# Attention, gated FFN and top-1 experts on one core: softmax steps reordered, PV in two runs, first FFN blocks between attention's last steps

## What is computed

```python
# attention: 4 batches x 8 heads, 576 tokens, head size 64, fp32
scores = 0.125 * q @ k.T                  # masked block-causally, blocks of 64 tokens
attn   = exp(scores - max) ; attn /= attn.sum(-1) + 1e-9
x = (attn @ v), heads side by side        # 2304 x 512
# gated FFN, 512 -> 1536 -> 512
y = (sigmoid(x @ w_gate) * (x @ w_val)) @ w_out
# top-1 of 8 experts, 512 -> 1024 -> 512
out[t] = gate[t] * relu(y[t] @ w1[e]) @ w2[e],  e = argmax(y[t] @ wr)
```

## Time and profile before

| | |
|---|---|
| median of 3 runs | 988.29 us (987.73 to 992.08) |
| profiled execution | 989.87 us, its span 988.2 us |
| busy | PE 914.9 us (93%), DVE 338.4 (34%), ACT 298.7 (30%), POOL 253.3 (26%) |
| attention stage | 5.3 us to 213.0 us; a pair takes about 12.6 us |
| mean granted TensorE clock | 0.973 of full speed |
| DMA sizes, median us from issue to landing | w1raw 768 KB, 5.5; kt and qt 288 KB each, 3.5 and 4.0; rwide 144 KB in two issues, 2.9; xo store 288 KB, 3.1; rinv store 4.5 KB, 2.7; xraw 768 KB, 4.6 |

### The profile page before, as it was taken

One profiled execution on the slowest core, in us unless ns is written; L12 is line 12 of the kernel. 1 busy time (PEld: TensorE's weight loads), 2 busy tenths in 40 slices (PEclk: granted clock), 3 DMA queues, 4 the chain that ended last, 5 costly groups with the idle time before them and its releaser, 6 DMA issues.

```text
span 988.2 us, 15746 instructions
## 1 busy us (share of the span) xinstructions
PE 914.9 (93%) x5370; PEld 758.9 (77%) x5371; DVE 338.4 (34%) x635; ACT 298.7 (30%) x654; POOL 253.3 (26%) x249
## 2 busy tenths in 40 slices
PE   6888888889999999999999999999379998999995
PEld 3444444469999999999999999998268887888884
DVE  5666666652210200210110120112663444235421
ACT  4555454433222212112112112112253354134310
POOL 4033333312211111111111111111444344225421
PEclk9999999999999999999999999999599999999998
DMA  4444444333110100000010000000373556116310
GB/s 131 152 153 153 136 135 147 124 122 107 43 43 33 33 1 32 6 27 32 1 32 32 1 1 11 23 2 32 138 260 132 190 181 226 42 43 220 114 42 29
DMA packets 45536, 83.08 MB, mean 84 GB/s; under 512 B 6831, under 2 KB 19119, under 8 KB 45488
## 3 DMA queue, kind: packets, MB, share of 16 engines
q1 hardware_dynamic: 39728, 67.21, 20.9%
q0 software_dynamic: 3360, 10.49, 3.1%
q10 hardware_dynamic: 2400, 4.72, 1.3%
HBM read 68.17 MB, written 14.75 MB: 84 GB/s over the span
## 4 chain that ended last, share of the span: by engine, by line
PE 85%; DVE 4%; issue 3%; POOL 2%; DMA 2%; ACT 2%; ACTq 0%; DVEq 0%; SPq 0%; POOLq 0%
PE bank L1163 22%; PE bank L1165 22%; PE bank L1164 22%; PE bank L1130 6%; PE bank L1103 5%; PE bank L1091 4%; DVE nmax L842 2%; PE bank L1300 2%; DMA stage<-in_we 2%; PE bank L1222 1%; POOL ew1l L368 1%; ACT prob L672 1%; PE bank L1213 1%; PE bank L1274 1%; DVE xo L821 1%
## 5 line engine op out<-in xcount | busy, mean ns | idle before, releaser
L1163 PE MATMUL bank<-xh,w1h 128*128 128x384 f32 x576 | 196.0, 340 | 0.0
L1165 PE MATMUL bank<-xh,w1l 128*128 128x384 f32 x576 | 193.2, 335 | 0.0
L1164 PE MATMUL bank<-xl,w1h 128*128 128x384 f32 x576 | 193.1, 335 | 0.0
L573 POOL TENSOR_TENSOR hl<-hraw,hh 128x384 fp32r<-128x384 f32 x72 | 77.2, 1072 | 399.1 <-ACT hh L701 399.1
L890 DVE TENSOR_TENSOR hraw<-sig,bank 128x384 f32<-128x384 f32 x72 | 39.9, 555 | 340.8 <-ACT sig L730 340.7
L730 ACT ACTIVATE sig<-bank 128x384 f32<-128x384 f32 x72 | 35.4, 492 | 259.5 <-PE bank L1165 259.5
L1163 PEld LDWEIGHTS bank<-xh,w1h 128*128 128x128 f32 x576 | 108.3, 188 | 1.8
L1164 PEld LDWEIGHTS bank<-xl,w1h 128*128 128x128 f32 x576 | 108.3, 188 | 1.7
L672 ACT ACTIVATE prob<-bank,nmax 128x576 f32<-128x576 f32 (+2 forms) x144 | 76.3, 531 | 105.5 <-DVE nmax L842 88.3
L1165 PEld LDWEIGHTS bank<-xh,w1l 128*128 128x128 f32 x576 | 108.1, 188 | 0.0
L1091 PE MATMUL bank<-kt,qt 64*64 64x64 f32 (+7 forms) x640 | 71.5, 441 | 16.6 <-ACT prob L672 11.3
(11 more groups left out here) (147 smaller groups left out, 1299.6 us busy)
## 6 DMA issues: line engine op xcount, KB each, us to landing
stage<-in_we SPq DMA_DIRECT2D x56, 512.0 KB
w1raw<-in_w SPq DMA_DIRECT2D x8, 768.0 KB, 5.5
kt<-in_kT SPq DMA_DIRECT2D x16, 288.0 KB, 3.5
qt<-in_qT SPq DMA_DIRECT2D x16, 288.0 KB, 4.0
rwide<-rinv_scratch SPq DMA_DIRECT2D x32, 144.0 KB, 2.9
xt_scratch<-xo SPq DMA_DIRECT2D x16, 288.0 KB, 3.1
xraw<-xt_scratch SPq DMA_DIRECT2D x6, 768.0 KB, 4.6
y_scratch<-yrow ACTq DMA_DIRECT2D x6, 768.0 KB, 3.6
```

The costliest lines, as they stand in the source:

```text
L573: pool.tensor_tensor(hl[:, f % 2, :], hraw[:, f % 2, :], hh[:, f % 2, :].bitcast(F32), ALU.subtract).then_inc(h_low, 1)
L1163: pe.matmul(out_, wh, ah, start=first, stop=False, skip_group_check=True)
L1164: pe.matmul(out_, wh, al, start=False, stop=False, skip_group_check=True)
L1165: return pe.matmul(out_, wl, ah, start=False, stop=last, skip_group_check=True)
```

## The change

1. **DVE's order in a pair.** Copies stand in a table (`OUT_V`). The maximum of step 0 comes ahead of the copy of the last pair's u6; the copy of u8 stays behind maximum 1; `recips` is one step earlier (step 1); `o_out` moves from step 1, where it did pair g-2, to step 8, where it does pair g-1.
2. **ACT's order** (`OUT_A`). The copy of the last pair's u9 comes ahead of exponential 2 and no longer behind it.
3. **PE.** PV's parts at steps 6 and 8 become one run at step 6.
4. **SP.** `o_store(g-2)` moves behind the v loads (ahead of `w1raw`); the first `xraw` load moves ahead of the last batch's pairs; the wait for the last `xo` store ahead of the `w_out` loads is gone.
5. **POOL** splits the first x in the last batch (`x_split`); ACT and DVE no longer do.
6. **Handover.** PE does `turn` of u6 and u7, then `up(0,0,0)`, then u8, u9, PV, and `up(0,0,1)`. The last `o_out` comes behind the first `hraw`. The last batch is written out behind the loop on all engines.

```diff
-        LAG, PE_LAG = 3, 4
+        PE_LAG = 4
+        OUT_V = {0: (1, 5), 1: (1, 7), 3: (0, 0), 4: (0, 1), 5: (0, 2), 6: (0, 3)}
+        OUT_A = {0: (1, 6), 2: (1, 8), 3: (0, 0), 7: (0, 4)}
-        PV_STEP = {4: [0], 6: [1, 2], 8: [3, 4]}
-        RSUM_STEP, O_STEP = 2, 1
+        PV_STEP = {4: [0], 6: [1, 2, 3, 4]}
+        RSUM_STEP, O_STEP = 1, 8
...
@@ SP, pair @@
                 if not early:
-                    if p == 3:
-                        o_store(b, 0)
-                    elif not isinstance(b, int):
-                        o_store(b - 1, p + 1)
                     rinv_store(g - 2, p % 2)
                     rwide_load(g - 2, p % 2)
                     sp.wait_ge(pv_done, g - 1)
...
+                if p >= 2:
+                    o_store(b, p - 2)
+                elif not (isinstance(b, int) and b == 0):
+                    o_store(b - 1, p + 2)
...
             xload(0, PPB)
-            o_store(BATCH - 1, PPB - 3)
+            for p in range(PPB):
+                pair(BATCH - 1, p)
...
-            o_store(BATCH - 1, PPB - 1)
             sp.wait_ge(pv_done, NPAIR)
-            sp.wait_ge(w1_low, 2 * C)
-            for i in range(2):
-                sp.wait_ge(xo_stored[i], 16 * NPAIR // 2)
+            sp.wait_ge(scores_done, NB * NPAIR)
             for k in range(FC):
+                if k == 2:
+                    o_store(BATCH - 1, PPB - 1)
...
@@ ACT, pair @@
+                    if i == 2 and not start:
+                        after_unit(g - 1, p - 1, OUT_A[i][1])
                     act.wait_ge(nmax_done, n + 1)
...
-                    if i >= LAG:
-                        after_unit(g, p, i - LAG)
-                    elif not start:
-                        after_unit(g - 1, p - 1, i + NB - LAG)
+                    if i != 2 and i in OUT_A and not (start and OUT_A[i][0]):
+                        back, j = OUT_A[i]
+                        after_unit(g - back, p - back, j)
...
@@ DVE, pair @@
+                    if i in OUT_V and not (start and OUT_V[i][0]):
+                        back, j = OUT_V[i]
+                        after_unit(g - back, p - back, j)
                     if i == RSUM_STEP and not start:
                         recips(g - 1, (p - 1) % 2)
...
-                    if i == O_STEP and not (isinstance(b, int) and g < 2):
-                        o_out(g - 2, p % 2)
+                    if i == O_STEP and not start:
+                        o_out(g - 1, (p - 1) % 2)
...
@@ PE, end of attention @@
+            turn(NPAIR - 1, PPB - 1, NB - 4)
+            turn(NPAIR - 1, PPB - 1, NB - 3)
+            pe.wait_ge(exp_done, NB * NPAIR - 2)
+            up(0, 0, 0)
+            turn(NPAIR - 1, PPB - 1, NB - 2)
+            turn(NPAIR - 1, PPB - 1, NB - 1)
+            pv(NPAIR - 1, PPB - 1, list(range(KT_N)))
+            pe.wait_ge(exp_done, NB * NPAIR)
+            up(0, 0, 1)
             group(0, 0)
```

More of the change, by code:

```diff
@@ L124, in bass_attention_ffn_moe @@
         wol = sb(s2, "wol", [P, FC, D], F32R)
+        woraw = sb(s2, "woraw", [P, 2, D])
         xh.append(sb(s2, "xh1", [P, C, GT], F32R))
         xl.append(sb(s2, "xl1", [P, C, GT], F32R))
-        woraw = sb(s2, "woraw", [P, 2, D])
         yrow = sb(s2, "yrow", [P, GM, D])
@@ L452, in _ @@
             sp.dma_start(wr_sb[:], wr.rearrange("(c p) e -> p c e", p=P)).then_inc(wr_loaded, 16)
-            with sp.Fori(1, BATCH) as b:
+            with sp.Fori(1, BATCH - 1) as b:
                 for p in range(PPB):
@@ L547, in w1_split, with x_split @@
                                    ALU.subtract).then_inc(w1_low, 1)
+            def x_split():
+                pool.wait_ge(x_loaded, 16)
+                pool.tensor_copy(xh[0][:].rearrange("p c n -> p (c n)"), xraw[:].rearrange("p c n -> p (c n)")
+                                 ).then_inc(x_high, 1)
+                pool.wait_ge(x_high, 1)
+                pool.tensor_tensor(xl[0][:].rearrange("p c n -> p (c n)"), xraw[:].rearrange("p c n -> p (c n)"),
+                                   xh[0][:].rearrange("p c n -> p (c n)").bitcast(F32), ALU.subtract
+                                   ).then_inc(x_low, 1)
             def pair(b, p):
@@ L557, in pair @@
                     w1_split(2 * b)
-                elif p == 0 and not isinstance(b, int):
+                elif p == 0 and not (isinstance(b, int) and b == 0):
                     w1_split(2 * b - 1)
+                elif p == 1 and isinstance(b, int) and b == BATCH - 1:
+                    x_split()
             for p in range(PPB):
                 pair(0, p)
-            with pool.Fori(1, BATCH) as b:
+            with pool.Fori(1, BATCH - 1) as b:
                 for p in range(PPB):
                     pair(b, p)
+            for p in range(PPB):
+                pair(BATCH - 1, p)
             w1_split(2 * C - 1)
@@ L674, in pair @@
                                    ).then_inc(exp_done, 1)
-                    if i >= LAG:
-                        after_unit(g, p, i - LAG)
-                    elif not start:
-                        after_unit(g - 1, p - 1, i + NB - LAG)
+                    if i != 2 and i in OUT_A and not (start and OUT_A[i][0]):
+                        back, j = OUT_A[i]
+                        after_unit(g - back, p - back, j)
             for p in range(PPB):
                 pair(0, p)
-            with act.Fori(1, BATCH) as b:
+            with act.Fori(1, BATCH - 1) as b:
                 for p in range(PPB):
                     pair(b, p)
+            for p in range(PPB):
+                pair(BATCH - 1, p)
             def xhigh(G, par):
@@ L689, in xhigh @@
                          ).then_inc(x_high, 1)
-            for i in range(NB - LAG, NB):
-                after_unit(NPAIR - 1, 1, i)
-            xhigh(0, 0)
+            after_unit(NPAIR - 1, 1, 6)
+            after_unit(NPAIR - 1, 1, 8)
             act.wait_ge(scores_done, NB * NPAIR)
@@ L843, in pair @@
                                       ).then_inc(nmax_done, 1)
+                    if i in OUT_V and not (start and OUT_V[i][0]):
+                        back, j = OUT_V[i]
+                        after_unit(g - back, p - back, j)
                     if i == RSUM_STEP and not start:
                         recips(g - 1, (p - 1) % 2)
[L846 to L849, removed]
-                    if i == O_STEP and not (isinstance(b, int) and g < 2):
-                        o_out(g - 2, p % 2)
+                    if i == O_STEP and not start:
+                        o_out(g - 1, (p - 1) % 2)
             for p in range(PPB):
                 pair(0, p)
-            with dve.Fori(1, BATCH) as b:
+            with dve.Fori(1, BATCH - 1) as b:
                 for p in range(PPB):
                     pair(b, p)
+            for p in range(PPB):
+                pair(BATCH - 1, p)
             def xlow(G, par):
@@ L861, in xlow @@
                 dve.tensor_tensor(xl[par][:], xraw[:], xh[par][:].bitcast(F32), ALU.subtract).then_inc(x_low, 1)
-            after_unit(NPAIR - 1, 1, NB - LAG)
-            after_unit(NPAIR - 1, 1, NB - LAG + 1)
-            o_out(NPAIR - 2, 0)
+            after_unit(NPAIR - 1, 1, 5)
             recips(NPAIR - 1, 1)
-            after_unit(NPAIR - 1, 1, NB - 1)
-            xlow(0, 0)
-            o_out(NPAIR - 1, 1)
+            after_unit(NPAIR - 1, 1, 7)
             def yT_evac(i, m, last=False):
@@ L890, in group @@
                     dve.tensor_tensor(hraw[:, f % 2, :], sig[:, f % 2, :], val_ps, ALU.mult).then_inc(hraw_done, 1)
+                    if first and f == 0:
+                        o_out(NPAIR - 1, 1)
                     if first:
@@ L1150, in _ @@
                 pair(0, p)
-            with pe.Fori(1, BATCH) as b:
+            with pe.Fori(1, BATCH - 1) as b:
                 for p in range(PPB):
                     pair(b, p)
[L1154 to L1159, removed]
+            for p in range(PPB):
+                pair(BATCH - 1, p)
             def three(out_, wh, wl, ah, al, first, last):
@@ L1228, in group @@
                 for f in range(FC):
-                    up(G, par, f)
+                    if not (first and f < 2):
+                        up(G, par, f)
                     if f >= 2:
```

## The result

| | before | after |
|---|---|---|
| median | 989.68 us (4 runs, 987.73 to 992.08) | 977.37 us (4 runs, 973.81 to 979.76) |
| after / before | | 0.987, 95% interval 0.985 to 0.990 |
| profiled execution, its span | 989.87, 988.2 us | 973.81, 972.1 us |
| exponential 0 of pair 1, of pair 15 | 18.02, 196.99 | 16.83, 186.31 |
| first `down` | 226.23 | 213.28 |

The change is 12.3 us (1.3%) faster by the medians. The prediction had 5.7 us. Of the 16.1 us between the two spans 12.95 are there at the first `down`. The other 3.1 come later, in code that the change doesn't touch. From the first `down` to the end of the span the fourteen traces of this document took 758.8 to 763.4 us (before 762.0, after 758.8, the least), so the 3.1 are spread.

The account below looks back on a forecast made before the run. PE's waits in attention, made by instruction order, were taken as the bound. Pairs -18.3, handover -1.0, refill stalls +11.2, xraw +2.4 sum to -5.7 us: 982.6 us from median 988.29, 8-in-10 range 968 to 994.

Parts of the forecast that it names:

- The reordered pair: Attention pair, T counted from its first score matmul S0: new order cuts 12.62 to 11.3 us; 18.3 us over all pairs.
- The late refill: Heads of even pairs: o_out waits 1.86 us for rwide behind w1raw; six times, 11.2 us lost.
- 7.6, the lower row: SP in w1raw pairs: rwide's read issued 7.6 us behind w1raw, the lower of rows 7.6 to 8.8.
- The `xraw` stall: Behind pair 11's w1raw: the first xraw load makes one refill stall 2.4 us longer, at most 2.9.
- The fixed cost of about 2.0 us: Read of rwide: the skill page's DMA cost would make o_out 0.4 late, sum about 9 us better; 3.5 used instead.
- Handover: From the last pair to the first down: down at T 18.4 instead of 19.4, 1.0 us gained, bounds 0 and 2.
- It is mostly the waits that move: Handover: the same PE work remains, so only 1.0 us is gained.
- In time: Rival, w1raw pairs: the small store slips through in 2.5 us, all 19.3 us stay, 969.0; chance 0.22.
- S1's chain: Rival, ahead of S1: chain S4 to exponential 8 is 0.6 longer in 15 pairs, about 989; chance 0.15.
- The long stall with a fall of the clock: Rival, pairs 4 to 14: o_out 3.1 late plus 1.5 for the clock each, 999.0; chance 0.15.
- the point of 2.8: Stalls at even pairs: from 2.8 us each on, the long-stall rival decides, the gain being used up.
- The sign: Whole kernel: faster by over 0.5% at chance 0.5, within 0.5% at 0.32, slower at 0.18.

Follow-up runs that it names:

- E1: Changed kernel with the w1raw load moved behind the next read of rwide; 967.41 us, 0.979 of the kernel before.
- E6: E5 with PV in three parts (steps 4, 6, 8), as in the kernel before; 965.67 us, 0.976 of the kernel before.
- E10: E9 with PV in three parts; 964.48 us, 0.974 of the kernel before.
- E2: Changed kernel with the first xraw load issued one pair later, behind SP's pair 12; 979.14 us, one run.
- E3: Changed kernel with the load moves of E1 and E2 together; 971.11 us, 0.983 of the kernel before.
- E11: Changed kernel with PE's old handover (four transposes, PV, then up for both blocks); 982.24 us, one run.
- E8: Kernel before with only the change's orders on DVE and ACT, o_out left in the pair after; 971.88 us, 0.981 of the kernel before.
- E12: E8 without DVE's addition of 1e-9 to the row sums; 970.37 us, 0.980 of the kernel before.
- E9: E5 without DVE's addition of 1e-9 to the row sums; 964.25 us, 0.974 of the kernel before.
- E7: Kernel before with one edit, ACT's copy of u9 ahead of exponential 2; 974.40 us, 0.983 of the kernel before.
- E5: Changed kernel with w1raw and the first xraw load each behind a read of rwide; 970.66 us, 0.980 of the kernel before.

## Why the prediction was right or wrong

Direction, range and mechanism held; the size was under half. The 13.0 below are those of two single executions, that of after its fastest; by the medians the forecast's 5.7 stands against 12.3 in all. For the chain up to the first `down`, with the prediction's terms turned to the stretches of the two traces:

| stretch | forecast | measured | where it differs |
|---|---|---|---|
| to exponential 0 of pair 1 | 0 | -1.2 | pair 0 gains too; the sum had no term (16.8 to 17.5 in the kernels with its order) |
| pairs 1 to 14, work | -17.0 | -19.8 | a pair is 11.15, not 11.3 |
| pairs 1 to 14, stalls | +13.6 | +10.8 | read issued 6.3 to 7.3 behind `w1raw`, not 7.6 |
| pairs 1 to 14, clock | 0 | -0.5 | two falls each, 3.0 before, 2.5 after |
| exponential 0 of pair 15 to `down` | -2.3 | -2.3 | |
| sum | -5.7 | -13.0 | |

**The reordered pair.** All the points held within 0.1: S1 at T 1.85 (1.94), its wait 0.29 (0.36), exponential 0 at 2.51 (2.54), S2 at 3.48 (3.52), `recips` ended at 4.53 (4.6), store at 4.63 (4.7), u1 without a wait. From S2 to the next S0 I left before's row as it was, less the 1.08: 7.74. It is 7.6, in E1's undisturbed pairs too; PV in one run seems to save it (argued from PE's rows, not shown: E6 and E10 have other waits in the place). Over 12 pairs that is 1.7 of the 2.8 us; 0.4 are pairs 1 and 2, which gained more than taken, and 0.5 that before's other pairs took 12.66 on the mean and not pair 14's 12.62.

**The late refill.** The mechanism is shown by E1: it is `w1raw`'s bytes, with those of k and q, ahead of the small store and read, at the heads of the even pairs, six times as forecast. The mis-sized term is the one I took as "7.6, the lower row". With T taken from S0, pair 9 has `w1raw` at 2.62 (2.63), the store at 4.80 (4.7), the read at 9.05 (10.25), `o_out` at 12.89 (13.75). The time from `w1raw` to the read was 6.3 to 7.3 (8.4 with `xraw`) and that from the read to the use 3.7 to 4.4, where I had 3.5. The two errors have opposite signs; a plain stall is 1.4 on average instead of 1.86. In the earlier trace rows the store was issued 4.4 behind `w1raw`, here 2.2 behind: the time to the read hangs on the store's own place too, and not on `w1raw`'s drain alone, as I had it (read from the rows; the place of the `xo` store changed with it). The `xraw` stall was 3.69 for 4.26, and E2 and E3 gave about 2 us for `xraw` alone, near the 2.4 taken. The fixed cost of about 2.0 us comes from a fit that the Trainium skill (DMA: Bandwidth & Descriptors, Anatomy of one DMA — SWDGE (gpsimd) path) gives for DMAs issued from GpSimd; the reads of `rwide` are issued from SP, and the fit adds a term for the bytes. They are two issues of 144 KB each, 288 KB in all, and not 144 KB in all as the table and the prediction have it. No read that DVE waited for in after came near 2.0 us, with 3.7 to 4.4 from issue to use.

**Handover.** -2.3 and T 18.4 were forecast and measured, but for half the reason. E11 has it that the order is worth 0.5 and the clock that it keeps 1.7; E8 and E12, with PV, `o_out` and handover as before, took 3 us longer than before and 5 longer than E9 here. "It is mostly the waits that move" was right for the order and blind to the clock; that the number fits is partly luck.

**The rivals.** In time: not so, though E1 is nearly that world (one stall of 1.5 us is left) and came out at 967.4 against the 969.0 worked out for it. S1's chain: it was 0.07 shorter, not 0.6 longer. The long stall with a fall of the clock: the fall did come behind two of six stalls and cost 1.3 each, but with the 1.4 of a plain stall the point of 2.8 was reached once only. **The sign** was safe: the six stalls cost 10.8 us of the some 24 that the rest gained, and would have had to be twice what they were.

**What I didn't see.** First, the gain is not spread over the edits: E7's one moved copy gives 1.7%, and the move of `o_out` to the pair's end, with PV in one run, brings nothing in the pairs (E12 against E9) while it creates the stalls. Secondly, the additions of DVE that wait for POOL, which cost more as soon as `w1raw` is moved (E5 against E9, 6.4 us).

## What to carry to other kernels

Read which waits the order of one in-order engine makes, and try the single smallest move first: here one copy of 0.27 us ahead of one exponential gave all that the six edits together gave (without the stalls and the addition they come to 2.6% against its 1.7%). When a consumer is moved earlier, follow its data back through every queue, and put bulk loads behind the small round trip that has a date, since a queue of its own gave it only 0.2 us. Then look at what the moved loads set going on other engines. When a stage is shortened, look at the next stage's head again, where a wait that was covered comes free and may take the clock with it.

## What the runs showed of the hardware

- **DVE and POOL.** A DVE addition from SBUF to SBUF of 128 x 9 elements took 0.165 us in the median and up to 3.11 (E5) and 2.57 (E3), ending with POOL's 3.44 us subtraction of two SBUF operands, while DVE's reciprocals next to it stayed at 0.17 to 0.19. POOL's 1.46 us cast, with one operand, holds it as well: 1.42 (E5), 1.33 (E6), 1.05 in the kernel before. Two additions that began together with or ahead of a subtraction took 0.16 (E1 at 166.08, E3 at 119.27). The Trainium skill (GPSIMD Engine Reference, Specifications) says that the two share SBUF interfaces, and contend when DVE is in a 2-port mode or has two SBUF inputs; that the wait lasts to the end of POOL's instruction is these rows'.
- **Small DMAs among large ones.** From a 4.5 KB store to the read issued when it had landed: in after 2.2 to 2.9 us with 576 KB (k and q) ahead, 4.1 to 4.6 with 768 KB more issued 2.2 to 2.9 us ahead, 6.15 with `xraw` besides; 2.9 with 768 KB but without k and q (2.2 to 4.7 in the other kernels); 5.8 behind `xraw`, k and q (E2). From a queue of its own 0.2 less on the mean, with the bulk or without. E9 has one of 4.1 with neither `w1raw` nor `xraw` issued in the 8 us ahead; its cause stays open.
- **The clock.** In attention the granted clock fell to its lower level (0.5 of full speed) in none to four places of a trace, each some 1.2 to 1.5 us; none in E1, E6 to E10 and E12, of which E7's PE still waits up to 1.0 us for an exponential in each pair. The same attention code fell twice in after and four times in E11. At the old handover with shortened pairs it fell in each of the four kernels that had it (E7, E8, E11, E12); the kernel before, with its longer pairs, kept it there.
